# First batch with its queries first and the norm weight spread by a product; steady batches with the next attention's quarters 2 + 1 + 2

## The reference

```python
# attention without softmax; q, k, v: [8, 8, 576, 64]
kv = einsum('bhsd,bhse->bhde', k, v)
out = einsum('bhsd,bhde->bhse', q, kv)
x = out / sqrt(mean(out * out, -1) + 1e-6) * g_norm      # heads side by side: x is [8, 576, 512]
# phase a, per batch
theta = x @ w_theta                                      # 512 x 512
y = w_tok_r @ (x * cos(theta)) + w_tok_i @ (x * sin(theta))   # 576 x 576 over the tokens
u = x + y
x2 = u + maximum(u @ w_ch, 0)
# phases b, c, d: a second mixer with w_tok1, w_tok2, w_ch1, w_ch2
```

## Time and profile before

| | us |
|---|---|
| median of 3 runs (lowest, highest) | 1176.63 (1175.86, 1177.12) |
| the profiled execution: time, span | 1176.91, 1175.1 |
| batch 0, until the first theta product of batch 1 | 103.3 |
| a steady batch (six of them) | 63.9 |
| PE busy in the span | 1154.3 |

### The profile page before, as it was taken

How to read it: one execution, slowest core, us unless ns; L and a number is a source line. 1 busy time by engine, 2 the same in 40 slices (tenths; PEclk the granted TensorE clock), 3 DMA queues, 4 the chain that set the end, 5 groups by cost and what they waited for, 6 DMA issues and landing times.

```text
span 1175.1 us, 20563 instructions
## 1 busy us (share of the span) xinstructions
PE 1154.3 (98%) x7790; PEld 1116.7 (95%) x7790; DVE 834.9 (71%) x1243; ACT 481.0 (41%) x758; POOL 327.9 (28%) x210
## 2 busy tenths in 40 slices
PE   5999999999999999999999999999999999999998
PEld 5799999999999999999988999999999999999998
DVE  3968878686969687777557667667666786666664
ACT  3623425141424233334343555555556543333331
POOL 4462434444353534331552313214200000000000
PEclk9999999999999999999999999999999999999999
DMA  9714526160625330319997888666768999999983
GB/s 278 197 28 107 122 69 133 44 144 13 164 38 149 52 80 0 83 42 303 332 310 279 280 310 272 266 238 242 286 229 312 397 300 293 262 252 307 296 207 54
DMA packets 327383, 228.25 MB, mean 194 GB/s; under 512 B 231440, under 2 KB 295312, under 8 KB 326288
## 3 DMA queue, kind: packets, MB, share of 16 engines
q1 hardware_dynamic: 324912, 227.03, 63.3%
q10 hardware_dynamic: 2400, 0.30, 0.2%
HBM read 136.84 MB, written 92.80 MB: 195 GB/s over the span
## 4 chain that ended last, share of the span: by engine, by line
PE 86%; DMA 5%; DVE 3%; SPq 2%; issue 1%; POOL 1%; ACT 1%; DVEq 0%; ACTq 0%; POOLq 0%
PE bank L43 10%; PE bank L45 10%; PE bank L44 10%; PE bank L1377 10%; PE bank L1379 10%; PE bank L1378 10%; PE bank L367 6%; PE bank L373 6%; PE bank L368 6%; DMA u_scratch<-attention_u 3%; PE bank L312 3%; PE bank L326 1%; PE bank L282 1%; DMA attention_g<-g_scratch 1%; DVE attention_u L1268 1%
## 5 line engine op out<-in xcount | busy, mean ns | idle before, releaser
L367 PE MATMUL bank<-weights_tok,z_z 128*128 128x288 f32 x576 | 164.3, 300 | 0.3
L368 PE MATMUL bank<-weights_tok,z_z 128*128 128x288 f32 x576 | 161.2, 294 | 0.0
L373 PE MATMUL bank<-weights_tok,z_z 128*128 128x288 f32 x576 | 125.0, 295 | 0.8 <-POOL z_z L965 0.6
L367 PEld LDWEIGHTS bank<-weights_tok,z_z 128*128 128x128 f32 x576 | 108.1, 188 | 1.2 <-issue 1.1
L368 PEld LDWEIGHTS bank<-weights_tok,z_z 128*128 128x128 f32 x576 | 108.1, 188 | 0.0
L948 POOL TENSOR_TENSOR weights_rms_inverse<-weights_mean_squares,weights_minus_half 128x8 f32<-128x8 f32 x40 | 66.4, 1662 | 114.2 <-DVE weights_mean_squares L725 114.0
L373 PEld LDWEIGHTS bank<-weights_tok,z_z 128*128 128x128 f32 x576 | 92.5, 187 | 1.3 <-POOL z_z L965 0.8
L596 ACT ACTIVATE weights_x_channel_major<-attention_u 128x288 fp32r<-128x288 f32 x64 | 28.5, 446 | 139.0 <-DVE attention_u L792 139.0
L43 PE MATMUL bank<-weights_x_channel_major,weights_ch 128*128 128x288 f32 x256 | 77.4, 302 | 0.0
L963 POOL TENSOR_TENSOR z_z<-tokens_cos,z_z 128x512 fp32r<-128x512 f32 x24 | 31.9, 1329 | 159.8 <-ACT z_z L589 143.8
L45 PE MATMUL bank<-weights_x_channel_major,weights_ch 128*128 128x288 f32 x256 | 75.4, 294 | 0.0
(11 more groups left out here) (297 smaller groups left out, 3589.7 us busy)
## 6 DMA issues: line engine op xcount, KB each, us to landing
g_scratch<-attention_staged SPq DMA_DIRECT2D x36, 960.0 KB, 3.9
weights_g<-g_scratch SPq DMA_DIRECT2D x24, 1152.0 KB, 10.6
g_scratch<-attention_staged SPq DMA_DIRECT2D x36, 384.0 KB, 4.7
x_scratch<-attention_u SPq DMA_DIRECT2D x8, 1152.0 KB, 4.5
u_scratch<-attention_u SPq DMA_DIRECT2D x16, 576.0 KB, 7.6
weights_raw_u<-u_scratch SPq DMA_DIRECT2D x6, 1536.0 KB, 7.7
qkv_u_left<-u_scratch SPq DMA_DIRECT2D x12, 768.0 KB, 10.1
x_tokens_scratch<-z_x_turned SPq DMA_DIRECT2D x112, 72.0 KB, 2.0
```

What stands on the lines that cost most here:

```text
L367: pe.matmul(out, x, wtok[0][:, zt, hs], start=(i == 0), stop=False)
L368: pe.matmul(out, x, wtok[1][:, zt, hs], start=False, stop=False)
L373: mm = pe.matmul(tok_bank(b, g)[:, 0:HALF], z[1][:, zt, c * P:(c + 1) * P], wtok[0][:, zt, half * HALF:(half + 1) * HALF], start=False, st ...
```

## The change

**Batch 0.** (1) The norm weight comes as one row of 256 B by a DMA from ACT's queue, PE multiplies a row of ones with it, and DVE copies the result. (2) SP issues all q tiles and w_theta ahead of w_tok_r and w_tok_i; w_ch comes in two halves after `g_zlo` reaches 6. (3) PE begins with 24 transposes of the identity, then does all five attends (five banks, no wait for norms but for the last), x transpose 0, and then theta 0 to 3 by parts, each with the next x transpose inside, and the twelve groups of token weights between and after them. (4) ACT makes the magnitudes (Abs) and the block diagonal of batch 1, which DVE did. (5) w_ch is split in two halves while token_mix runs its groups.

**Steady batches.** Attends 0 and 1 both stand after pair 3, attend 2 after group 4, attends 3 and 4 after group 7; x transposes 0 and 1 both after channel_mix 6. ACT's squares and DVE's mean squares and norms follow that order.

```diff
+
+    ps_out_first = [*ps_out, ps_acc[0], ps_acc[1], ps_out[0]]
+
+
+    ps_wt = [ps_acc[i % 2] for i in range(9)] + [ps_out[0], ps_acc[2], ps_acc[1]]
+
+    def out_bank(n, j):
+        return ps_out_first[j] if isinstance(n, int) and n == 0 else ps_out[j % 2]
+
     def tok_bank(b, g):
...
         load_left(vin, v, 0, s_kv0[2])
-        sp.dma_start(gn[:, :], g_norm.rearrange("(a d) -> a d", a=1).broadcast_to([P, D])).then_inc(s_raw[1], DMA)
         for j in range(NT):
             load_query_tile(0, j, s_q0[j])
-            if j == 1:
-                load_tok(w_tok_r, raw_tok[0], s_raw[3])
         sp.dma_start(raw_theta[:, :, :], w_theta.rearrange("(c p) n -> p c n", p=P)).then_inc(s_raw[0], DMA)
+        load_tok(w_tok_r, raw_tok[0], s_raw[3])
         load_tok(w_tok_i, raw_tok[1], s_raw[4])
-        sp.dma_start(raw_ch[:, :, :], w_ch.rearrange("(c p) n -> p c n", p=P)).then_inc(s_raw[2], DMA)
         load_kv(1)
         sp.wait_ge(p_qt, NT)
         for j in range(NT):
             load_query_tile(1, j, s_q)
 
-        def body(b):
+        def load_ch():
+
+            sp.wait_ge(g_zlo, 6)
+            for part in range(2):
+                rs = slice(part * DM // 2, (part + 1) * DM // 2)
+                sp.dma_start(raw_ch[part][:, :, :], w_ch[rs, :].rearrange("(c p) n -> p c n", p=P)).then_inc(s_ch[part], DMA)
+
+        def body(b, first=False):
             load_kv(b + 2)
+            if first:
+                load_ch()
             load_blocks(b + 2)
             store(b)
             for c in range(NC):
                 store_turned(sp, b, c, turned[c])
...
-            wait(pe, d_xn, NT * n + max(j - 1, 0))
+            if isinstance(n, int) and n == 0:
+                if j == NT - 1:
+                    pe.wait_ge(d_xn, 1)
+            else:
+                wait(pe, d_xn, NT * n + max(j - 1, 0))
             if j == 1:
                 wait(pe, d_turns, n)
             for hp in range(HP):
-                mm = pe.matmul(ps_out[j % 2][0:rows(j), hp * P:(hp + 1) * P], qt[:, hp, j * P:j * P + rows(j)],
+                mm = pe.matmul(out_bank(n, j)[0:rows(j), hp * P:(hp + 1) * P], qt[:, hp, j * P:j * P + rows(j)],
                                kvbd[hp // 2][:, hp % 2, :], start=True, stop=True)
             mm.then_inc(p_out, 1)
...
                 for w, x in ((0, 0), (0, 1), (1, 0)):
-                    if x == 0:
-                        pe.wait_ge(*((a_whi, 2) if w == 0 else (d_wlo, 2)))
-                    else:
-                        pe.wait_ge(d_xlo, 1)
+                    if x == 1:
+                        pe.wait_ge(d_xlo, j + 1)
                     for c in range(NC):
-                        mm = pe.matmul(ps_theta[0][:, :], xcm[x][:, c * S:c * S + P], wth[w][:, c, :],
+                        if x == 0 and c % 2 == 0:
+                            pe.wait_ge(*((a_whi, c // 2 + 1) if w == 0 else (d_wlo, c // 2 + 1)))
+                        mm = pe.matmul(ps_theta[j][:, :], xcm[x][:, c * S + j * P:c * S + (j + 1) * P], wth[w][:, c, :],
                                        start=(w == 0 and x == 0 and c == 0), stop=(w == 1 and c == NC - 1))
+                    if w == 0 and x == 0:
+                        x_transpose(b, j + 1)
                 mm.then_inc(p_theta, 1)
                 return
...
+                if first and pair == NT - 1:
+                    pe.wait_ge(a_whi, 3)
+                    pe.wait_ge(d_wt, 2 * NT + 1)
                 token_mix_pair(b, pair, FIRST_HALF)
                 if pair == (1 if first else NJ - 1):
                     attend(b + 1, 0)
+                if pair == NJ - 1 and not first:
+                    attend(b + 1, 1)
 
         def token_mix(b, g):
...
+        pe.wait_ge(s_ident, 2)
+        for i in range(24):
+            pe.transpose(ps_acc[0][:, 0:P], ident[:, :], ident[:, :])
+
+        pe.wait_ge(s_ident, 3)
+        pe.wait_ge(s_raw[1], NORM_LOADED)
+        pe.matmul(ps_acc[1][:, 0:D], ones[0:1, :], gn_row[0:1, :], start=True, stop=True).then_inc(s_raw[1], 1)
         pe.wait_ge(s_zero, 2)
         kv(0)
-        pe.wait_ge(s_ident, 2)
+        pe.wait_ge(s_raw[1], NORM_COPIED)
 
         q_transpose(0, 0)
         q_transpose(0, 1)
         attend(0, 0)
         attend(0, 1)
-        for j in range(2, NT):
-            tok_weight(2 * j - 4)
-            tok_weight(2 * j - 3)
-            q_transpose(0, j)
-            if j < NT - 1:
-                attend(0, j)
+        q_transpose(0, 2)
+        q_transpose(0, 3)
+        attend(0, 2)
+        q_transpose(0, 4)
+        attend(0, 3)
+        attend(0, 4)
         x_transpose(0, 0)
-        attend(0, NT - 1)
-        for j in range(NT):
-            if j + 1 < NT:
-                x_transpose(0, j + 1)
-            theta(0, j, by_parts=(j == 0))
-            tok_weight(NT + 1 + j)
-        tok_weight(2 * NT + 1)
+        theta(0, 0, by_parts=True)
+        tok_weight(0)
+        theta(0, 1, by_parts=True)
+        tok_weight(1)
+        tok_weight(2)
+        theta(0, 2, by_parts=True)
+        tok_weight(3)
+        tok_weight(4)
+        theta(0, 3, by_parts=True)
+        tok_weight(5)
+        tok_weight(6)
+        theta(0, 4)
+        tok_weight(7)
+        tok_weight(8)
+        tok_weight(9)
+        tok_weight(10)
+        tok_weight(11)
+        kv(1)
+        q_transpose(1, 0)
 
         def body(b, first=False, more=True):
             if not first:
                 for j in range(NT):
                     theta(b, j)
-            if more:
+            if more and not first:
                 kv(b + 1)
-                if first:
-                    q_transpose(b + 1, 0)
             if first:
-                pe.wait_ge(a_whi, 3)
                 pe.wait_ge(a_wt, 2 * NT)
-                pe.wait_ge(d_wt, 2 * NT + 1)
+                pe.wait_ge(a_left, 4)
+                pe.wait_ge(d_wt, 2 * NT)
             if more:
                 token_mix_first_half(b, first)
                 if first:
                     q_transpose(b + 1, 1)
                 for g in range(NC, NG):
                     token_mix(b, g)
-                    attend(b + 1, g - 3)
-                    if first and g < NG - 1:
-                        q_transpose(b + 1, g - 2)
+                    if first:
+                        attend(b + 1, g - 3)
+                        if g < NG - 1:
+                            q_transpose(b + 1, g - 2)
+                    elif g == NC:
+                        attend(b + 1, 2)
+                    elif g == NG - 1:
+                        attend(b + 1, 3)
+                        attend(b + 1, 4)
             else:
                 token_mix_last()
             if first:
-                pe.wait_ge(d_wlo, 3)
+                pe.wait_ge(d_wlo, 4)
             for g in range(NG):
                 channel_mix(b, g)
-                if more and g == 4:
+                if more and g == 6:
...
-            act.wait_ge(d_abs, NT * b + j + 1)
+            if isinstance(b, int) and b == 0:
+                act.activation(cos_tile[j][0:m, :], frac[0:m, i, :], ACT.Abs).then_inc(a_abs, 1)
+                act.wait_ge(a_abs, j + 1)
+            else:
+                act.wait_ge(d_abs, NT * (b - 1) + j + 1)
             act.activation(cos_tile[j][0:m, :], cos_tile[j][0:m, :], ACT.Sin, scale=-TWO_PI,
                            bias=half_pi[0:m, :]).then_inc(a_sin, 1)
...
+                if not first:
+                    squares(b + 1, 1)
+            if first:
+                ch_weight_hi(0)
             for g in range(NG):
                 u_hi(b, g)
+                if first and g == 2:
+                    ch_weight_hi(1)
+                if more and not first and g == NC:
+                    squares(b + 1, 2)
                 if first and g == 0:
                     q_copy(b + 1, 1)
-                if more and g >= NC:
+                if first and g >= NC:
                     squares(b + 1, g - 3)
-                    if first and g < NG - 1:
+                    if g < NG - 1:
                         q_copy(b + 1, g - 2)
+            if more and not first:
+                squares(b + 1, 3)
+                squares(b + 1, 4)
...
-                        magnitude(0, j)
-                    if j == NJ:
-                        fraction(0, 3)
-                        magnitude(0, 3)
-                    tok_weight_lo(NT + 1 + j)
-                tok_weight_lo(2 * NT + 1)
+                tok_weight_lo(0)
+                fraction(0, 0)
+                magnitude(0, 0)
+                x_lo(0, 2)
+                norm(0, 4)
+                tok_weight_lo(1)
+                tok_weight_lo(2)
+                fraction(0, 1)
+                magnitude(0, 1)
+                x_lo(0, 3)
+                tok_weight_lo(3)
+                tok_weight_lo(4)
+                fraction(0, 2)
+                magnitude(0, 2)
+                x_lo(0, 4)
+                tok_weight_lo(6)
+                fraction(0, 3)
+                magnitude(0, 3)
```

(31 more changed lines are left out.)

149 lines of the change are left out of this document (81 added, 68 removed).

## The result

The changed kernel takes 1182.52 us (median of 6 runs, 1180.89 to 1184.72), the kernel before 1176.71 beside it (6 runs): a ratio of 1.0053, interval [1.0043, 1.0063]. It is slower by 5 to 7 us, over the 1181.5 at which my range ended. The profiled execution is the quickest of the six, 1180.89 us with a span of 1179.1, that is 4.0 over the profiled one of before, so the trace has to explain 4.0 us, and the remaining 1.8 us of the 5.8 between the medians lie in the other executions. One execution of the whole study, one of rest_first, took 1263.60 us at a mean granted clock of 0.85 and is left out of its figures.

The account below looks back on a forecast made before the run. TensorE was taken to bound the steady batches, w_theta's landing and then GpSimd the first. Terms: -4.6 (first batch) - 1.0 (switches) + 6.9 (wait for norm 0) = +1.3, so 1178.2 us, 1177.9 against the median; range 1172.5 to 1181.5.

Parts of the forecast that it names:

- (a): First batch, loads: w_tok_r behind w_theta and a one-row norm weight let theta's weight land at 21.1 us instead of 25.1.
- (b): First batch, work before theta reordered, all five attends first: token_mix starts at 48.3 us instead of 51.68, 3.4 us won.
- (c): First half of token_mix, batch 0: earlier z_lo and a moved w_ch split bring 15.4 us instead of 16.52, 1.2 won.
- Rival 4: First half of token_mix: POOL and DVE block each other, the half takes 16.5 us again, 1179.0 us in all; chance 0.10.
- The w_ch split: Batch 0: moved to later token_mix groups, where DVE stands idle 1.75 us in each before a norm.
- Steady batches: Six batches: joined switches win 0.15 us each, but attend 2 waits for norm 0, about 1.15 us each, 6.9 lost.
- (d): 24 transposes ahead of kv(0): kv(0) may end 1.3 us earlier, mostly hidden; only 0.5 us remains, inside (b).
- -4.6: First batch in all: 4.6 us won from the earlier token_mix start and shorter first half, bounds 2.5 and 7.
- +5.9: Rest of the sum: 1.0 us won by joined switches, 6.9 us lost by the wait for norm 0.
- Rival 2: Start of batch 0 bound by DVE and ACT passing banks: token_mix at 50.3 us, 1180.5 us in all; chance 0.27.

Follow-up runs that it names:

- rest_first: norm_early with, in batch 0, the left rows' fraction ahead of rotate 3 and each w_ch split half ahead of the mean square: 1173.63 us, ratio 0.9983.
- short_rotates: norm_early without warming, w_ch split halves ahead of the mean square, rotates 2 and 3 of batch 0 on 8 columns instead of 512: 1173.03 us, one execution.
- dve_lo: norm_early without warming, w_ch split halves ahead of the mean square, three of nine low parts of batch 0 on VectorE: 1173.15 us, ratio 0.9975.
- no_warm: The changed kernel without the 24 transposes ahead of kv(0): 1181.91 us, ratio 1.0049 to the kernel before.
- start_only: The changed kernel with all edits of batches 1 to 6 taken back, new first batch kept: 1174.69 us, ratio 0.9992 [0.9981, 1.0002].
- norm_early: The changed kernel with norm 0 of a steady batch after residual 1 instead of residual 2 on VectorE: 1174.68 us, ratio 0.9982.
- steady_only: The kernel before with only the order of batches 1 to 6 changed: 1183.54 us, ratio 1.0061.
- before_warm: The kernel before with only the 24 transposes ahead of kv(0) added: 1177.35 us, ratio 1.0014.

## Why the prediction was wrong

- **(a) and (b), the work before token_mix: right.** w_theta was there at 21.22 us (I had 21.1), theta's first products stand at 23.08 (23.4) and the first token product at 48.04 (48.3). The one inner mark that was off is the end of norm 3, at 29.13: I had 28.3, and the terms as I wrote them add up to 28.05.
- **(c), the first half: wrong, the step that failed first.** "I count 15.4 us for the half" took GpSimd's low parts as free once they could start earlier. The half stayed at 16.56, so the 1.2 us that I booked (1.12 by my own figures) were not won. Rival 4 had this mechanism and its price, 16.5 us, and the earlier trace rows showed it, 1.77 us for a rotate that takes 0.68. What I did not do is add up: nine low parts at 1.25 and eight two-tile operations of VectorE at 0.6 are 16.1 us, more than TensorE's 15.1. With that sum rival 4 would have been my own course, and not a chance of 0.10. short_rotates and dve_lo show that this work is what bound it. The sum is a rough measure and no exact time: in the changed kernel GpSimd also stands idle for 2.01 us before its last low part, until ScalarE's high part of the last tile is there, and rest_first shows that taking that wait away alone wins nothing. The rule of the Trainium skill ("SBUF — State Buffer", shared port pair) agrees with the traces to within 0.14 us: 1.70 us for one of each, against 1.24 + 0.60 = 1.84 if one stood wholly behind the other.
- **The w_ch split: I costed its new place at nothing** because VectorE idles there before a norm. That idle time is the wait for GpSimd's power, and the split made the power 2.54 us long instead of 1.64. The price was 0.45 us, shown by rest_first, whose edit gave it back.
- **Steady batches: right in mechanism, near in size.** The pause costs 1.18 us a batch (I had 1.15) and the joins bring 0.09 (I had 0.15), which is 1.09 net against 1.00, or 0.5 us over six batches.
- **(d), warming.** It did bring the fast pace to kv(0), 36 ns a product against 59. The rule of the Trainium skill that transposes do not count for the clock gate ("TensorE: Matmul & The Clock Gate", Part 4) is not what these traces show; they list the 24 as f32 matmuls with the identity, and whether these run in the transpose mode that the page means they do not tell. The 0.35 us that it brings in the quick executions (no_warm's theta at 100.28 against 99.93) does not show in the medians, which are level with and without it.
- **The sum.** My -4.6 for the first batch became -3.15: 1.24 us were missing in the half and 0.45 through the split, and (b) won 0.24 more than I had. My +5.9 became +6.54. That makes +3.4 in place of +1.3, or 1180.3 against 1176.9 where I had 1178.2; the last stores add the 0.6 us up to 1180.89. The other error is as large, and is in the step from the profiled execution to the median: I took 0.28 us off for the runs, but here the profiled run was the quickest of six, 1.6 us under the median. Of the 4.6 us between my 1177.9 and the measured 1182.5, 2.1 are in the terms, 0.6 in the stores and 1.9 in this step. The new start can lose 2.1 us in an execution. The profiles of start_only and norm_early show this; for the changed kernel itself only the clocks of 0.996 to 0.998 speak for it, since both its profiles have the good start, so how much of the 1.9 us it accounts for is not shown. Before, w_theta's landing hid most of that: steady_only, whose first batch is the old one, had the slow start too (attends at 1.06 us), and its first steady theta came only 0.15 us later.
- **Rival 2** gave 1180.5 and is the nearest in number, but not in mechanism: VectorE and ScalarE passed banks as fast as laid out. Nor does its number follow from its condition: with the start at 50.3 the first batch still wins 2.6 us and not 2.0.
- **The range** ended at 1181.5 since I cut both ends of 1171 to 1182.5; a scatter that the new start brings with it had no place in it.

Left open: what decides, from one execution to the next, when TensorE's fast pace comes and whether it holds, how much of the changed kernel's scatter comes from that, and why TensorE waits for up to 3.6 us on stores in phase b in some.

## What to carry to other kernels

When an operation is moved ahead of others on its engine, ask which result behind it someone waits for, and by how much its turn moves: here one norm, 0.9 us late in a place without slack, made a gain of some 2 us into a loss of 6, and moving it by one step brought all of it back. Where two engines hold each other up, add the durations of both and compare the sum with the time of the engine that should be the bound; an idle stretch of one engine is no free place if it is the other's working time. And when a change takes away a wait that covered others, like a start that waits for a transfer, count the scatter that the wait had hidden.

## What the runs showed of the hardware

- GpSimd's operation on 128x8 values takes 1.64 us alone and 2.54 beside a 1.22 us subtraction of two SBUF tiles on VectorE, which is not longer for it (1.22 also in rest_first, with no power beside it). There the subtraction came first, by 0.18 us. When the two engines follow each other without a gap, both show it: low parts of 1.74 instead of 1.28 and rotates of 1.78 instead of 0.68.
- The granted clock of the profile reads 1.00 at the very beginning although the products run at half pace (an attend's four in 1.06 us). In these traces a fall shows, as 0.50, only after TensorE has once been at full pace (start_only, norm_early, rest_first, before_warm). The durations of like products are the thing to read there.
- Two groups of four f32 products side by side cost the same as apart: attends 0 and 1 joined take 1.70 us and a single one 0.81, each with 0.08 more for getting back to the token products, so 1.78 against twice 0.89. All joins together give 0.09 us in a batch of 64.
